# Sum of squares through Gram matrices in a fused attention and two-layer network kernel

## The chip, the cores and the metric

The kernel runs on one core of one Trainium2 chip. The metric is the time of one execution on the device in microseconds, the median of three runs: 1582.67 us before the change (1582.47 to 1583.47).

## What is computed

Three stages follow one another, all in float32.

```
p_packed = sm_attn(p, k, v)                    # 32 packed rows per head attend to 576 keys
attn     = sm_attn(q, p_packed, p_packed)      # 576 tokens per head attend to the 32 packed rows
x        = attn as (4608 tokens, 512)
rms      = sqrt(mean(x * x, axis=-1) + 1e-6);  xn = x / rms * rms_g
y        = (silu(xn @ w_gate) * (xn @ w_val)) @ w_out          # 512 -> 1536 -> 512
out      = prelu(y @ w_in, alpha) @ w_out2                     # 512 -> 2048 -> 512
```

There are 8 batches with 8 heads of 64 dimensions. A token's row of x has 512 numbers, 64 from each head; what the change concerns is the mean of their squares.

## The kernel before

**Two large stages.** Stage A does the attention and the first layer, one batch after another, each in two halves of 288 tokens; stage B does the second layer in nine tiles of 512 tokens. Every main product is written as three passes (high by high, low by high, high by low part), on operands split into a high part that TensorE multiplies quickly (fp32r) and a rest.

**The fold.** x is never built for the first layer. The probabilities a2 (32 packed rows of four heads on 128 partitions, times two groups e, times 288 tokens) are multiplied with m, the packed values already multiplied into the gate and value weights. Making m for a batch takes six "folds" (`folded`, L709): products of the packed values with the weights into two PSUM banks, whose high part ScalarE copies out (m_hi, L937) and whose rest VectorE subtracts (m_lo, L1146). In the first batch some folds go through a raw copy (L931) and GpSimd splits them (`split_m`, L502).

**The norm.** The root of the mean square is needed per token. The kernel before builds x for it: `tokens_out` (L649) has four groups x0 to x3 per batch, two for each half, each of four matmuls in 32x64 tiles of the array (L673), writing two banks. ScalarE squares a group out of PSUM (L909). In the first batch four accumulating products with a constant matrix give the mean (L682); in the other batches GpSimd adds the four squares (L484, L486) and one product per half gives it (L688). VectorE copies the mean out and adds epsilon (L1116), ScalarE takes logarithm and exponential (`rsqrt`, L912, which loads a table first, and the following silu loads another), VectorE does a Newton step of three instructions (L1124 to L1129), and a2 is multiplied with the result (`normed`, GpSimd; in the first batch `normed0`, VectorE). The two halves do this one after the other. `split` then makes an_hi and an_lo from a2.

**The order.** A half of a batch on TensorE is a loop over 12 chunks f of 128 hidden units: gate product (6 matmuls), value product (6), and, two chunks behind, `down` (12). Gate and value have one PSUM bank each, so the gate of f+1 waits for silu of f (ScalarE, L972), the value of f+1 for the product of f (VectorE, L1188); h_hi (ScalarE, L978) and h_lo (VectorE, L1191) feed `down`. All work for the batch that comes next lies between these: three tables PE_PLACES, DVE_PLACES and ACT_PLACES say at which (half, place, f) each piece stands in the fixed order of its engine. The places of TensorE are "ready" (ahead of the last three matmuls of value f; waits of the piece are put here), "after" (behind value f), "ready_down" (ahead of the last three of `down`) and "between" (behind `down`). On the other engines they are "within" (ahead of the product of f), "after" (behind it) and "between" (behind h_hi or h_lo). The tables *_FIRST hold what is left of batch 0 and runs in the first half tile. Banks 2 and 3 are shared by scores, x groups, means and folds in the batches from 1 on, so each of them waits until the one before it has been read.

**The start.** Before the first tile the pieces of batch 0 run in the order of a list at the end of each engine's program, with filler products (`keep_busy`, L804) that write nothing of use where TensorE would stand still. SP issues the loads: gv (four blocks, gate and value weights) and ow (three blocks, the output weights).

Of the kernel before, what the change touches and what calls it, by code (L numbers as in the profile page):

```python
# [73 lines left out]
}  # L74
PE_FIRST = {
    (0, "after", 3): ["x2"], (0, "between", 3): ["x3"], (0, "between", 4): ["mean1"],
# [3 lines left out]
    (0, "within", 5): ["mean1"], (0, "between", 7): ["newton1", "normed1"], (0, "within", 10): ["split1"],  # L80
}
ACT_FIRST = {
    (0, "after", 0): ["fold5"], (0, "after", 3): ["x2"], (0, "between", 3): ["x3"],
    (0, "between", 6): ["rsqrt1"], (0, "within", 9): ["split1"],
# [4 lines left out]
           "fold5": (1, LATE_BANK)}  # L89
# [4 lines left out]
def build(nc, q_t, k_t, v_s, p_t, w1_gv, w1_o, w2, rms_g, alpha, out_t):  # L94
# [3 lines left out]
    with ExitStack() as ctx:  # L98
# [42 lines left out]
        newton = place("newton", [P, HALF])  # L141
# [98 lines left out]
        def sq_of(c):  # L240
            return sq_0 if first(c) else sq
# [13 lines left out]
        def mean_ps(c, h):  # L255

            return psum[:, 1 if first(c) and h == 0 else 3, 0:HALF]

        def x_bank(c, i):

            return 0 if first(c) and i == 0 else 2

        def m_bank(c, j):

            return [4, 6, 4, 6, 2, 4][j] if first(c) else 2
# [41 lines left out]
        s2_mm, x_mm, mean_mm, m_mm = sem("s2_mm"), sem("x_mm"), sem("mean_mm"), sem("m_mm")  # L307
# [9 lines left out]
        squared, sq_part, mean_copied = sem("squared"), sem("sq_part"), sem("mean_copied")  # L317
# [39 lines left out]
        def _(sp):  # L357
# [96 lines left out]
        def _(pool):  # L454
# [7 lines left out]
            pool.wait_ge(consts_set, 3)  # L462
            nc.gpsimd.memset(v_sb[0:LAST, CHUNKS - 1, :], 0.0).then_inc(consts_set, 1)
# [17 lines left out]
            def squares(c, h):  # L481
                n = 4 * (c - 1) + 2 * h
                pool.wait_ge(squared, 4 * c + 2 * h + 2)
                nc.gpsimd.tensor_tensor(sq[:, 0:2, :], sq[:, 0:2, :], sq[:, 2:4, :], ALU.add).then_inc(sq_part, 1)  # L484
                pool.wait_ge(sq_part, n + 1)
                nc.gpsimd.tensor_tensor(sq[:, 0, :], sq[:, 0, :], sq[:, 1, :], ALU.add).then_inc(sq_part, 1)  # L486

            def normed(c, h):
                pool.wait_ge(newton_step, 6 * c + 3 * h + 3)
                nc.gpsimd.tensor_tensor(a2[:, h], a2[:, h], rinv[:, h, :].unsqueeze(1).to_broadcast([P, GROUPS, HALF]),  # L490
                                        ALU.mult).then_inc(a2n_done, 1)
# [10 lines left out]
            def split_m(j):  # L502

                n = SPLIT_BY_POOL[j]
                blocks = slice(2 * j, 2 * j + 2)
                pool.wait_ge(m_raw_done, n)
                nc.gpsimd.tensor_copy(m_hi[:, blocks], m_raw[:, blocks]).then_inc(m_part, 1)
                pool.wait_ge(m_part, n)
                nc.gpsimd.tensor_tensor(m_lo[:, blocks], m_raw[:, blocks], m_hi[:, blocks].bitcast(F32),
                                        ALU.subtract).then_inc(m_split, 1)  # L510
# [20 lines left out]
            for c in range(1, BATCH):  # L531
                scaled(c)
                squares(c, 0)
                normed(c, 0)
                squares(c, 1)
                normed(c, 1)
# [27 lines left out]
        def _(pe):  # L564
# [6 lines left out]
            def scores_ready(c, h):  # L571

                pe.wait_ge(k_in[h], 16 * (c + 1))
                if h == 0:
                    pe.wait_ge(p_in, 16 * (c + 1))
                    if c == 1:

                        pe.wait_ge(m_raw_done, 2)
                    elif c > 1:
                        pe.wait_ge(mean_copied, 2 * c)  # L580
# [50 lines left out]
            def tokens_ready(c, h):  # L631
# [4 lines left out]
                else:  # L636
                    pe.wait_ge(s2_turned, 4 * c + 2)

            def tokens(c, h):

                q = q0_sb if first(c) else q_sb
                for pair in range(PAIRS):
# [6 lines left out]
            def tokens_out(c, i):  # L649

                h = i // 2
                if i % 2 == 0:
                    pe.wait_ge(a2_turned, 2 * c + h + 1)
                if first(c):
                    if i == 1:
                        pe.wait_ge(s2_turned, 4)
                    if i == 2:
                        pe.wait_ge(scores_out, 2)
                    if i == 3:
                        pe.wait_ge(squared, 3)  # L660
                elif i == 0:
                    pe.wait_ge(m_lo_done, evicted(c) + 2)
                elif i == 1:
                    pe.wait_ge(m_lo_done, evicted(c) + 4)
                elif i == 2:
                    pe.wait_ge(mean_copied, 2 * c + 1)
                else:
                    pe.wait_ge(m_lo_done, evicted(c) + 8)
                for k in range(2):
                    pair = 2 * (i % 2) + k  # L670
                    keys = slice(PACK * pair, PACK * (pair + 1))
                    for e in range(2):
                        mm = nc.tensor.matmul(psum[HEAD_DIM * e:HEAD_DIM * (e + 1), x_bank(c, i) + k, 0:HALF],  # L673
                                              pp[keys, e, :], a2[keys, h, e, :], start=True, stop=True)
                mm.then_inc(x_mm, 1)

            def mean(c, h):

                if first(c):
                    for pair in range(PAIRS):  # L680
                        pe.wait_ge(squared, 1 + pair // 2 if h == 0 else 4)
                        mm = nc.tensor.matmul(mean_ps(c, h), mean_w[:], sq_0[:, pair, :], start=pair == 0,  # L682
                                              stop=pair == PAIRS - 1)
                    mm.then_inc(mean_mm, 1)
                else:
                    pe.wait_ge(m_lo_done, evicted(c) + 6 + 4 * h)
                    pe.wait_ge(sq_part, 4 * (c - 1) + 2 * h + 2)
                    nc.tensor.matmul(mean_ps(c, h), mean_w[:], sq[:, 0, :], start=True, stop=True).then_inc(mean_mm, 1)  # L688

            def fold_ready(c, j):  # L690
# [3 lines left out]
                if first(c):  # L694
                    pe.wait_ge(gv_in[(2 * j + 1) * W1_GROUPS // NF1], 16)
                    if j in (2, 3):
                        pe.wait_ge(m_lo_done, 2 * (j - 1))
                    if j == 4:
                        pe.wait_ge(squared, 2)
# [4 lines left out]
                elif j < 5:  # L704
                    pe.wait_ge(squared, 4 * c + j)
                else:
                    pe.wait_ge(mean_copied, 2 * c + 2)
# [12 lines left out]
            def beside(c, name):  # L720
# [17 lines left out]
                if name[0] == "x":  # L738
                    tokens_out(c, int(name[1:]))
                if name in ("mean0", "mean1"):  # L740
                    mean(c, int(name[-1]))
                if name[:4] == "fold":
# [17 lines left out]
            def tile(b, half, at):  # L760
                n = 2 * b + half
                for f in range(NF1 + LAG):
                    if f < NF1:
                        if f == 0:
                            pe.wait_ge(an_lo_done, n + 1)
                        if half == 0 and b == 0 and f // 2 in SPLIT_BY_POOL:
                            pe.wait_ge(m_split, SPLIT_BY_POOL[f // 2])
# [21 lines left out]
                    if f >= LAG:  # L789
                        d = f - LAG  # L790
                        if n == 0 and d == 0:
                            pe.wait_ge(m_lo_done, 2 * len(SPLIT_AS_USUAL))
                            pe.wait_ge(m_raw_done, len(SPLIT_BY_POOL))
# [468 lines left out]
```

## Time and profile before

| | |
|---|---|
| median of three runs | 1582.67 us |
| profiled execution | 1583.42 us, span 1581.6 us |
| TensorE busy | 1561.9 us (99%) |
| VectorE, ScalarE, GpSimd busy | 733.2, 487.4, 211.4 us |
| mean granted clock | 0.998 of full speed |

The span runs from the first to the last instruction of the profiled execution. A matmul's row shows start and duration; matmuls are pipelined, so what one costs is the distance between starts and not its duration. A product in plain float32 appears as two rows (two passes), so x16 of a group means eight matmuls. Stage A fills the first half of the span, stage B the rest.

### The profile page before, as it was taken

Reading aid. Unit: us, or ns where it says so; the run is one execution under the profiler, and the core shown is the slowest. Engines: PE = TensorE matmul, PEld = TensorE weight load, DVE = VectorE, ACT = ScalarE, POOL = GpSimd, SP = SyncE. Lnnn points to the kernel's source line nnn. Section 1 sums busy time; section 2 is a strip of 40 time slices with the busy share of each in tenths; the row PEclk is TensorE's granted clock in tenths of the full one; section 3 lists DMA queues with packets and bytes.
Section 4 is the critical chain, followed back from the end, with each engine's and each line's share of the span. In section 5 each row is a group of like instructions: output and inputs, shape, how many; then the busy total and the mean of one; then the engine's idle time right before and its main releaser. Section 6 shows DMA issues by size and latency. Waiting matters only on the chain.

```text
span 1581.6 us, 25864 instructions
## 1 busy us (share of the span) xinstructions
PE 1561.9 (99%) x10396; PEld 1319.7 (83%) x10396; DVE 733.2 (46%) x1259; ACT 487.4 (31%) x909; POOL 211.4 (13%) x149
## 2 busy tenths in 40 slices
PE   8999999999999999999999999999999999999998
PEld 3888889888897988889988888888888888888887
DVE  4655544545545455454553434343433434343343
ACT  4446354554544546352211111111111111111111
POOL 2611010000101001015570101010100101010000
PEclk9999999999999999999999999999999999999999
DMA  9212103021120212003120101010000001010000
GB/s 353 75 43 78 46 1 108 16 78 46 49 73 4 77 46 76 16 1 148 55 110 0 53 0 53 0 53 0 27 27 27 27 0 53 0 53 0 27 1 27
DMA packets 42739, 76.18 MB, mean 48 GB/s; under 512 B 2208, under 2 KB 19616, under 8 KB 42656
## 3 DMA queue, kind: packets, MB, share of 16 engines
q1 hardware_dynamic: 37472, 65.55, 12.1%
q10 hardware_dynamic: 5184, 9.44, 1.5%
q8 instruction: 62, 1.02, 0.3%
q14 instruction: 21, 0.17, 0.0%
HBM read 56.11 MB, written 18.87 MB: 47 GB/s over the span
## 4 chain that ended last, share of the span: by engine, by line
PE 93%; DVE 4%; ACT 1%; issue 1%; ACTq 0%; POOL 0%; DVEq 0%; POOLq 0%
PE psum L567 29%; PE psum L568 28%; PE psum L569 28%; PE psum L715 2%; PE psum L673 1%; DVE h_lo L1191 1%; DVE act_sb L1188 1%; PE psum L591 1%; PE psum L807 1%; ACT h_hi L978 1%; DVE m_lo L1146 1%; PE psum L605 1%; PE psum L620 1%; PE psum L645 1%; PE psum L688 0%
## 5 line engine op out<-in xcount | busy, mean ns | idle before, releaser
L1224 DVE TENSOR_TENSOR h_lo<-g,h_hi 128x512 fp32r<-128x512 f32 x144 | 126.7, 880 | 450.9 <-ACT h_hi L1005 450.9
L1005 ACT CAST h_hi<-g 128x512 fp32r<-128x512 f32 x144 | 89.4, 621 | 637.2 <-PE psum L569 566.5
L567 PE MATMUL psum<-an_hi,m_hi 128*128 128x288 f32 x768 | 236.8, 308 | 4.7 <-DVE act_sb L1188 4.5
L567 PE MATMUL psum<-h_hi,ow_hi 128*128 128x288 f32 x768 | 236.1, 307 | 0.9 <-DVE h_lo L1191 0.9
L568 PE MATMUL psum<-h_hi,ow_lo 128*128 128x288 f32 x768 | 227.2, 296 | 0.0
L568 PE MATMUL psum<-an_hi,m_lo 128*128 128x288 f32 x768 | 226.7, 295 | 0.0
L569 PE MATMUL psum<-h_lo,ow_hi 128*128 128x288 f32 x768 | 225.8, 294 | 0.0
L569 PE MATMUL psum<-an_lo,m_hi 128*128 128x288 f32 x768 | 225.7, 294 | 0.0
L567 PEld LDWEIGHTS psum<-an_hi,m_hi 128*128 128x128 f32 x768 | 144.0, 187 | 38.5 <-issue 28.5
L567 PEld LDWEIGHTS psum<-h_hi,ow_hi 128*128 128x128 f32 x768 | 144.1, 188 | 36.3 <-issue 34.6
L1188 DVE TENSOR_TENSOR act_sb<-act_sb,psum 128x288 f32<-128x288 f32 x192 | 86.8, 452 | 180.3 <-PE psum L569 170.6
L1191 DVE TENSOR_TENSOR h_lo<-act_sb,h_hi 128x288 fp32r<-128x288 f32 x192 | 107.2, 559 | 101.3 <-ACT h_hi L978 100.7
L568 PEld LDWEIGHTS psum<-h_hi,ow_lo 128*128 128x128 f32 x768 | 144.6, 188 | 0.4
L568 PEld LDWEIGHTS psum<-an_hi,m_lo 128*128 128x128 f32 x768 | 144.4, 188 | 0.4
L569 PEld LDWEIGHTS psum<-h_lo,ow_hi 128*128 128x128 f32 x768 | 144.5, 188 | 0.0
L569 PEld LDWEIGHTS psum<-an_lo,m_hi 128*128 128x128 f32 x768 | 144.3, 188 | 0.0
L567 PE MATMUL psum<-xs,w_hi_front 128*128 (+1 forms) x360 | 140.1, 389 | 0.5 <-ACT y_sb L988 0.5
L567 PE MATMUL psum<-h_hi,w_hi_front 128*128 128x512 f32 x360 | 140.6, 391 | 0.0
L568 PE MATMUL psum<-h_hi,w_lo_front 128*128 128x512 f32 x360 | 140.1, 389 | 0.0
L569 PE MATMUL psum<-h_lo,w_hi_front 128*128 128x512 f32 x360 | 140.1, 389 | 0.0
L569 PE MATMUL psum<-xs,w_hi_front 128*128 (+1 forms) x360 | 140.0, 389 | 0.0
L568 PE MATMUL psum<-xs,w_lo_front 128*128 (+1 forms) x360 | 140.0, 389 | 0.0
(137 smaller groups left out, 2428.8 us busy)
## 6 DMA issues: line engine op xcount, KB each, us to landing
k_sb<-k_t SPq DMA_DIRECT2D x16, 576.0 KB, 5.0
q_sb<-q_t SPq DMA_DIRECT2D x8, 1152.0 KB, 6.3
y_mid<-y_sb SPq DMA_DIRECT2D x16, 576.0 KB, 3.5
xs_raw<-y_mid SPq DMA_DIRECT2D x9, 1024.0 KB, 5.2
out_t<-o_sb ACTq DMA_DIRECT2D x36, 256.0 KB, 2.0
v_sb<-v_s SPq DMA_DIRECT2D x8, 1024.0 KB, 6.6
gv_sb<-w_gv SPq DMA_DIRECT2D x4, 1536.0 KB, 18.7
w_raw_front<-w SPq DMA_DIRECT2D x2, 2560.0 KB, 13.0
```

The costliest lines, as they stand in the source:

```text
L567: nc.tensor.matmul(dst, w_hi, hi, start=start, stop=False)
L568: nc.tensor.matmul(dst, w_lo, hi, start=False, stop=False)
L569: return nc.tensor.matmul(dst, w_hi, lo, start=False, stop=stop)
L591: mm = nc.tensor.matmul(dst, p_sb[dims, pair, :], k_sb[dims, pair, h * HALF:(h + 1) * HALF], start=True, stop=True)
L605: mm = nc.tensor.transpose(at_ps(c, t)[:, at:at + P], a_sb[:, g, KEY_STARTS[j]:KEY_STARTS[j] + P], ident[:])
L620: mm = nc.tensor.matmul(pp_ps[PACK * pair:PACK * (pair + 1), e * HEAD_DIM:(e + 1) * HEAD_DIM], a_t[:, j, col:col + PACK], v_sb[:, j, head ...
L645: mm = nc.tensor.matmul(s2_ps(e)[PACK * pair:PACK * (pair + 1), :], pp_t[dims, pair, :], q[dims, pair, h * HALF:(h + 1) * HALF], start=Tru ...
L715: mm = nc.tensor.matmul(psum[keys, m_bank(c, j) + e, :].rearrange("p (f n) -> p f n", f=2), pp_tg[dims, pair, :], gv_sb[dims, 2 * j:2 * j ...
L1005: nc.scalar.copy(h2_hi[:, f % 2, :], g32[:, f % 2, :]).then_inc(g_hi_done, 1)
L1188: nc.vector.tensor_tensor(act_sb[:, s, :], act_sb[:, s, :], val_ps, ALU.mult).then_inc(h32_done, 1)
L1191: nc.vector.tensor_tensor(h_lo[:, s, :], act_sb[:, s, :], h_hi[:, s, :].bitcast(F32), ALU.subtract).then_inc(h_lo_done, 1)
L1224: nc.vector.tensor_tensor(h2_lo[:, s, :], g32[:, s, :], h2_hi[:, s, :].bitcast(F32), ALU.subtract).then_inc(g_lo_done, 1)
```

## The change

The mean square of a token is a quadratic form of its probabilities: for each head, a' G a with G the 32x32 product of the packed values with themselves. The change computes these Gram matrices (eight small matmuls per batch, ahead of the token scores), VectorE multiplies them with a mask `own` that keeps the blocks of a head (`gram`), TensorE multiplies the block matrix with a2 in full-size products (v, two per half), VectorE multiplies v with a2 and adds the two groups (`weigh`), and one product with the constant matrix per half gives the mean. The two means, the root and the Newton step of both halves are done together in batches 1 to 7. ScalarE's squares and GpSimd's additions go. Folds 2 to 5 move to other places. At the start the last gv block is loaded ahead of the first ow block, fold4 of batch 0 moves into the first tile, GpSimd splits raw folds in two pieces each, and there are fillers ahead of fold1 and gram0.

```diff
 PE_PLACES = {
-    (1, "ready", 1): ["fold0_ready"], (1, "after", 1): ["fold0"], (1, "between", 2): ["x0"],
-    (1, "ready", 3): ["fold1_ready"], (1, "after", 3): ["fold1"], (1, "between", 4): ["x1"],
-    (1, "ready", 5): ["fold2_ready"], (1, "after", 5): ["fold2"], (1, "between", 6): ["mean0"],
-    (1, "after", 7): ["x2"], (1, "ready_down", 7): ["fold3_ready"], (1, "between", 7): ["fold3"],
-    (1, "after", 9): ["x3"], (1, "ready_down", 9): ["fold4_ready"], (1, "between", 9): ["fold4"],
-    (1, "after", 11): ["mean1"], (1, "ready_down", 11): ["fold5_ready"], (1, "between", 11): ["fold5"],
+    (1, "ready", 1): ["fold0_ready"], (1, "after", 1): ["fold0"], (1, "between", 2): ["gram0"],
+    (1, "ready", 3): ["fold1_ready"], (1, "after", 3): ["fold1"], (1, "between", 4): ["gram1"],
+    (1, "between", 5): ["means"], (1, "ready_down", 6): ["fold2_ready"], (1, "between", 6): ["fold2"],
+    (1, "ready", 8): ["fold3_ready"], (1, "after", 8): ["fold3"],
+    (1, "ready", 10): ["fold4_ready"], (1, "after", 10): ["fold4"],
+    (1, "ready_down", 11): ["fold5_ready"], (1, "between", 11): ["fold5"],
 DVE_PLACES = {
-    (0, "between", 8): ["turn_s0"], (0, "after", 9): ["shift0"], (0, "between", 9): ["turn_s1"],
+    (0, "between", 8): ["turn_s0", "gram"], (0, "after", 9): ["shift0"], (0, "between", 9): ["turn_s1"],
-    (1, "between", 2): ["sums1"], (1, "after", 3): ["probs1"], (1, "between", 3): ["fold1"],
-    (1, "after", 4): ["turn_p1"],
+    (1, "between", 2): ["sums1", "weigh0"], (1, "after", 3): ["probs1"], (1, "between", 3): ["fold1"],
+    (1, "after", 4): ["turn_p1"], (1, "between", 4): ["weigh1"],
+    (1, "within", 6): ["means"], (1, "between", 6): ["fold2"], (1, "between", 7): ["newton"],
 ACT_PLACES = {
+    (1, "between", 1): ["fold0"], (1, "between", 3): ["fold1"], (1, "after", 6): ["rsqrt"], (1, "between", 6): ["fold2"],
+    (1, "between", 8): ["fold3"], (1, "between", 9): ["split0"], (1, "between", 10): ["fold4"], (1, "between", 11): ["fold5"],
 PE_FIRST = {
-    (0, "after", 3): ["x2"], (0, "between", 3): ["x3"], (0, "between", 4): ["mean1"],
+    (0, "ready", 0): ["fold4_ready"], (0, "after", 0): ["fold4"], (0, "after", 3): ["gram1"], (0, "after", 4): ["mean1"],
 DVE_FIRST = {
+    (0, "between", 3): ["weigh1"], (0, "within", 5): ["mean1"], (0, "between", 7): ["newton1", "normed1"],
...
+           "fold1": (2, LATE_BANK), "gram0": (1, LATE_BANK), "fold5": (1, LATE_BANK)}
...
-            for n in range(W1_GROUPS - 1):
+            for n in range(W1_GROUPS):
                 load_gv(n)
             load_ow(0)
-            load_gv(W1_GROUPS - 1)
...
             def tokens(c, h):
+                if h == 0:
+                    for pair in range(PAIRS):
+                        for e in range(2):
+                            dims = slice(HEAD_DIM * e, HEAD_DIM * (e + 1))
+                            mm = nc.tensor.matmul(psum[PACK * pair:PACK * (pair + 1), 2 + e, HALF:HALF + PACK],
+                                                  pp_t[dims, pair, :], pp_t[dims, pair, :], start=True, stop=True)
+                    mm.then_inc(gram_mm, 1)
...
+            def gram(c, h):                                   # TensorE
+                pe.wait_ge(a2_turned, 2 * c + h + 1)
+                if first(c) and h == 1:
+                    pe.wait_ge(scores_out, 2)
+                elif not first(c):
+                    pe.wait_ge(m_lo_done, evicted(c) + 2 + 2 * h)
+                for e in range(2):
+                    mm = nc.tensor.matmul(psum[:, gram_bank(c, h) + e, 0:HALF], gram_sb[:, e, :], a2[:, h, e, :],
+                                          start=True, stop=True)
+                mm.then_inc(v_mm, 1)
...
             def fold_ready(c, j):
+                elif j == 1:
+                    pe.wait_ge(weighed, 2 * c + 1)
+                elif j == 2:
+                    pe.wait_ge(mean_copied, 2 * c + 2)
                 else:
-                    pe.wait_ge(mean_copied, 2 * c + 2)
+                    pe.wait_ge(m_lo_done, evicted(c) + 2 * j)
...
+            def gram(c):                                      # VectorE
+                dve.wait_ge(gram_mm, c + 1)
+                reached(dve, v_mm, 2 * c)
+                for e in range(2):
+                    within = psum[:, 2 + e, HALF:HALF + PACK].unsqueeze(1).to_broadcast([P, PAIRS, PACK])
+                    nc.vector.tensor_tensor(gram_sb[:, e, :].rearrange("p (q k) -> p q k", q=PAIRS), within, own[:],
+                                            ALU.mult).then_inc(gram_set, 1)
+            def weigh(c, h):
+                n = 2 * c + h + 1
+                w, bank = sq_of(c)[:, h], gram_bank(c, h)
+                dve.wait_ge(v_mm, n)
+                nc.vector.tensor_tensor(w, psum[:, bank:bank + 2, 0:HALF], a2[:, h], ALU.mult).then_inc(weighed, 1)
+                dve.wait_ge(weighed, n)
+                nc.vector.tensor_tensor(w[:, 0, :], w[:, 0, :], w[:, 1, :], ALU.add).then_inc(w_summed, 1)
```

## Rows read from the trace of the kernel before

**Rows 1.** The page: busy time of each engine, granted clock in 40 slices.
```profile
PE 1561.9 (99%) x10396; PEld 1319.7 (83%) x10396; DVE 733.2 (46%) x1259; ACT 487.4 (31%) x909; POOL 211.4 (13%) x149
...
PEclk9999999999999999999999999999999999999999
```
**Rows 2.** TensorE's waits from 75 to 1040 us: total, times, longest.
```profile
PE psum L567 <- DVE act_sb L1188: 3.4, 9, 1.2
PE psum L673 <- DVE m_lo L1146: 1.8, 7, 0.3
```
**Rows 3.** Timeline around an x group: start, duration, instruction.
```profile
106.03 0.29 PE L569 MATMUL psum<-h_lo,ow_hi 128*128 128x288 f32 x1
106.25 0.71 PE L673 MATMUL psum<-a,pp 32*64 32x288 f32 x8
...
107.13 0.29 PE L568 MATMUL psum<-an_hi,m_lo 128*128 128x288 f32 x1
```
**Rows 4.** Timeline around a mean product.
```profile
114.46 0.30 PE L569 MATMUL psum<-h_lo,ow_hi 128*128 128x288 f32 x1
114.60 0.65 PE L688 MATMUL psum<-sq,mean_w 128*128 128x288 f32 x2
...
115.21 0.29 PE L568 MATMUL psum<-an_hi,m_lo 128*128 128x288 f32 x1
```
**Rows 5.** TensorE at the start: the packed values' products.
```profile
15.40 1.32 PE L620 MATMUL psum<-v_sb,a_t 128*32 128x64 f32 x80
```
**Rows 6.** VectorE in batch 2's preparation, half 1, f=2 to 3.
```profile
191.87 1.25 DVE L1146 TENSOR_TENSOR m_lo<-psum,m_hi 128x512 fp32r<-128x512 f32 x2
193.04 0.44 DVE L1188 TENSOR_TENSOR act_sb<-act_sb,psum 128x288 f32<-128x288 f32 x1
...
195.34 0.27 DVE L1100 RECIPROCAL rcp<-sum 128x18 f32<-128x18 f32 x1
...
196.25 0.75 DVE L1105 TENSOR_TENSOR e<-e,rcp 128x576 f32<-128x576 f32 x1
```
**Rows 7.** TensorE in batch 2's preparation: x0 to the fold's ready point in value 3.
```profile
193.27 0.71 PE L673 MATMUL psum<-a,pp 32*64 32x288 f32 x8 [0.26 <-DVE m_lo L1146]
...
195.21 0.29 PE L567 MATMUL psum<-an_hi,m_hi 128*128 128x288 f32 x1
```
**Rows 8.** ScalarE around one half's root.
```profile
215.99 1.06 ACT L937 CAST m_hi<-psum 128x512 fp32r<-128x512 f32 x2
217.06 1.28 ACT L972 ACT_TABLE_LOAD   x1
```
**Rows 9.** The start: VectorE and TensorE.
```profile
16.79 0.29 DVE L1070 COPY pp<-psum 128x128 f32<-128x128 f32 x1 [1.67 <-PE psum L620]
...
25.60 1.27 PE L673 MATMUL psum<-a,pp 32*64 32x288 f32 x16 [1.61 <-DVE a L1110]
...
27.60 3.91 PE L682 MATMUL psum<-sq,mean_w 128*128 128x288 f32 x8 [0.74 <-ACT sq L909]
...
31.55 0.46 DVE L1116 TENSOR_SCALAR mean<-psum 128x288 f32<-128x288 f32 x1 [3.58 <-PE psum L682]
...
36.78 0.40 PE L567 MATMUL psum<-an_hi,m_hi 128*128 128x288 f32 x1
```
**Rows 10.** Busy time per engine (PE, PEld, DVE, ACT, POOL), clock, DMA, GB/s.
```profile
20.00:25.00 5.00, 2.06 (x40) 0.37 (x32) 4.79 (x10) 2.55 (x5) 0.00 (x0) 0.93 1.01 404
25.00:27.00 2.00, 1.27 (x16) 0.34 (x16) 2.00 (x4) 0.27 (x2) 0.65 (x1) 0.50 1.04 390
```
**Rows 11.** First tile: ScalarE, GpSimd, VectorE, TensorE.
```profile
47.49 0.65 ACT L909 ACTIVATE sq<-psum 128x576 f32<-128x576 f32 x1 [0.71 <-PE psum L673]
...
53.89 2.46 POOL L509 TENSOR_TENSOR m_lo<-m_raw,m_hi 128x1024 fp32r<-128x1024 f32 x1
...
54.42 2.24 DVE L1058 TENSOR_SCALAR a_sb<-a_sb,rcp 128x576 f32<-128x576 f32 x1
...
59.32 0.85 PE L605 MATMUL psum<-ident,a_sb 128*128 128x128 f32 x6 [1.18 <-DVE mean L1116]
```

More of the change, by code:

```diff
@@ L140, in build @@
         a2 = place("a2", [P, 2, GROUPS, HALF])
-        newton = place("newton", [P, HALF])
+        gram_sb = place("gram_sb", [P, 2, P])
+        own = place("own", [P, PAIRS, PACK])
         p_sb = place("p_sb", [P, PAIRS, PACK])
@@ L240, in sq_of @@
         def sq_of(c):
-            return sq_0 if first(c) else sq
+            return (sq_0 if first(c) else sq)[:].rearrange("p (h e) n -> p h e n", e=2)
         def mean_of(c):
@@ L647, in tokens @@
                 mm.then_inc(s2_mm, 1)
[L649 to L675, printed above, removed]
@@ L690, in fold_ready @@
+            def mean(c, h):
+                pe.wait_ge(w_summed, 2 * c + (h + 1 if first(c) else 2))
+                nc.tensor.matmul(mean_ps(c, h), mean_w[:], sq_of(c)[:, h, 0, :], start=True, stop=True).then_inc(mean_mm, 1)
             def fold_ready(c, j):
@@ L737, in beside @@
                     tokens(c, int(name[-1]))
-                if name[0] == "x":
-                    tokens_out(c, int(name[1:]))
+                if name in ("gram0", "gram1"):
+                    gram(c, int(name[-1]))
                 if name in ("mean0", "mean1"):
                     mean(c, int(name[-1]))
+                if name == "means":
+                    mean(c, 0)
+                    mean(c, 1)
                 if name[:4] == "fold":
@@ L811, in _ @@
             for name in ("scores0", "scores1", "turn_a01", "turn_a2", "packed", "turn_packed", "tokens0", "fold0", "tokens1",
-                         "fold1", "x0", "x1", "mean0", "fold2", "fold3", "fold4", "fold5"):
+                         "fold1", "gram0", "mean0", "fold2", "fold3", "fold5"):
                 if name in FILLERS:
@@ L927, in folded @@
             def folded(c, j):
-                act.wait_ge(m_mm, NF1 // 2 * c + j + 1)
-                if first(c) and j in SPLIT_BY_POOL:
+                act.wait_ge(m_mm, FIRST_M[j] if first(c) else NF1 // 2 * c + j + 1)
+                if first(c) and j in RAW_M:
                     bank = m_bank(c, j)
@@ L991, in _ @@
             nc.scalar.preload_act_table_set("natural_log_exp_and_others")
-            for name in ("exp0", "exp1", "turn_a0", "turn_a2", "packed", "probs0", "fold0", "fold1", "x0", "x1", "probs1",
-                         "rsqrt0", "silu", "fold2", "split0", "fold3", "fold4"):
+            for name in ("exp0", "exp1", "turn_a0", "turn_a2", "packed", "probs0", "fold0", "fold1", "probs1",
+                         "rsqrt0", "silu", "fold2", "split0", "fold3", "fold5"):
                 beside(0, name)
@@ new lines, in weigh, with mean @@
+            def weigh(c, h):
[5 more added lines that the diff above has]
+                nc.vector.tensor_tensor(w[:, 0, :], w[:, 0, :], w[:, 1, :], ALU.add).then_inc(w_summed, 1)
+            def mean(c, halves):
+                dve.wait_ge(mean_mm, 2 * c + halves.stop)
+                if first(c):
+                    src = mean_ps(c, halves.start).unsqueeze(1)
+                else:
+                    dve.wait_ge(a2_turned, 2 * c + 2)
+                    src = psum[:, 2:4, 0:HALF]
+                nc.vector.tensor_scalar(mean_of(c)[:, halves, :], src, 0.0, RMS_EPS, ALU.max,
+                                        ALU.add).then_inc(mean_copied, halves.stop - halves.start)
@@ L1122, in newton_of @@
+            def newton_of(c, halves):
+                n = 3 * halves.start if first(c) else 3 * c + 3
+                root, whole, part = rinv_of(c)[:, halves, :], mean_of(c)[:, halves, :], sq_of(c)[:, halves, 1, :]
                 reached(dve, newton_step, n)
-                dve.wait_ge(rsqrt_done, 2 * c + h + 1)
-                nc.vector.scalar_tensor_tensor(out=newton[:], in0=mean_of(c)[:, h, :], scalar=-0.5, in1=root,
+                dve.wait_ge(rsqrt_done, n // 3 + 1)
+                nc.vector.scalar_tensor_tensor(out=part, in0=whole, scalar=-0.5, in1=root,
@@ L1169, in beside @@
                     turn_p(c, int(name[-1]))
+                if name == "gram":
+                    gram(c)
+                if name in ("weigh0", "weigh1"):
+                    weigh(c, int(name[-1]))
                 if name in ("mean0", "mean1"):
-                    mean(c, int(name[-1]))
+                    mean(c, slice(int(name[-1]), int(name[-1]) + 1))
+                if name == "means":
+                    mean(c, slice(0, 2))
                 if name in ("newton0", "newton1"):
-                    newton_of(c, int(name[-1]))
+                    newton_of(c, slice(int(name[-1]), int(name[-1]) + 1))
+                if name == "newton":
+                    newton_of(c, slice(0, 2))
                 if name in ("split0", "split1"):
@@ L1202, in _ @@
             dve.wait_ge(consts_set, 4)
-            for name in ("max0", "max1", "norm0", "norm1", "turn_a1", "packed", "turn_s0", "shift0", "turn_s1", "sums0",
-                         "probs0", "turn_p0", "shift1", "fold0", "fold1e0", "mean0", "fold1e1", "newton0", "normed0",
-                         "split0"):
+            for name in ("max0", "max1", "norm0", "norm1", "turn_a1", "packed", "turn_s0", "gram", "shift0", "turn_s1",
+                         "sums0", "probs0", "turn_p0", "shift1", "weigh0", "fold0e0", "mean0", "fold0e1", "newton0",
+                         "normed0", "fold1e0", "split0", "fold1e1"):
                 beside(0, name)
```

127 lines of the change are left out of this document (50 added, 77 removed), and 6 rows, old and new, of tables (ACT_PLACES, DVE_PLACES).

## The prediction

> **What bounds the kernel now.** I read the page's first two parts first: TensorE is busy for 99% of the span and its granted clock is at full speed in all forty slices [rows 1]. So the time is TensorE's instruction stream, and an edit is worth what it takes out of that stream or out of TensorE's waits. The waits come second: between 75 and 1040 us, in 965 us, TensorE idles 3.4 us for the gate-times-value product and 1.8 us for the first fold's low part; the second is 0.26 us in each of seven batches [rows 2]. No shorter wait in those 965 us can give much. The removed work must be found in the timeline, and every added wait must be looked for there.
>
> **The change in the steady batches (1 to 7).** They are alike, so I work out one and multiply by seven. Before, each has four x groups of four tiled matmuls, and two mean products.
> An x group: the last ordinary matmul ahead of it starts at 106.03, the second one behind it at 107.13. Without the group these would be two steps of 0.13 us apart, so a group costs 1.10 - 0.26 = 0.84 us [rows 3]. A full 128x128 f32 product over 288 columns: 114.46 to 115.21 less two steps is 0.48 us [rows 4]. The two mean products only move next to each other: 0.96 before and after.
> Removed: groups x2 and x3, 2 x 0.84 = -1.68. Groups x0 and x1 become two full products each, 0.96 for 0.84: +0.12 each. By TensorE work alone that is -1.44 a batch, -10.1 us in all.
> Tiny Gram products: eight matmuls of 32 columns, two passes each, in the tile shape of the token scores that follow them. The nearest row has 80 passes of 64 columns in 1.32 us, 0.0165 each [rows 5]: 16 x 0.0165 = 0.26. Issue and columns may hide behind the scores that follow in the same shape, so 0.05 is the lower end (a fifth of that), 0.40 the upper (half as much again). I take 0.2. The Trainium skill's page "TensorE: Matmul & The Clock Gate", section "Part 1: The HAM clock gate", says that starts of successive matmuls are never nearer than about 25 ns however few columns they have. By that rule the group takes 0.40 us and seven batches 1.4 us more than by my value; the 80 passes of [rows 5] are nearer together than that, so the row decides.
>
> **The wait that it adds.** In half 1 fold1 writes banks 2 and 3, in which v0 now lies, so fold1 must wait until VectorE has weighed v0. Before, ScalarE read x0 at once and this wait was free. VectorE is a strict chain here: low part of fold0 until 193.12, product of f=2, low part of h, the sums, whose reciprocal ends at 195.34 + 0.27 = 195.61, and only then the product of f=3 [rows 6]. The change puts weigh0 behind the sums. It is a 128x576 product with one operand in PSUM; a 128x576 one takes 0.75, a 128x288 one from PSUM 0.44 [rows 6], so 0.75, and "weighed" comes at 196.37. This moment doesn't depend on TensorE.
> TensorE: x0 waits for the low part and starts at 193.27, and the matmul behind the fold's ready point starts at 195.21 [rows 7]. Between them lie x0 (0.84 less the 0.10 lead) and nine matmuls, 0.13 apart. With v0: 193.27 + 0.96 + 9 x 0.13 = 195.4. The weighing releases it at 196.37, and a released group starts 0.15 later (193.12 to 193.27): 196.52. So there is a **new wait of some 1.1 us**, and this mark moves by 196.52 - 195.21 = +1.31, v0's own +0.12 being in it.
> Behind the waiting matmul stand the second half of value 3, fold1, down1; all move with it. VectorE adds the two rows (0.44) inside that time and is then waiting for TensorE, as now.
> Batch: +1.31 (x0 to v0 with the wait) + 0.12 (v1) - 1.68 (x2, x3) + 0.2 (Gram) = **-0.05 us**, seven batches -0.35. Bounds: weigh0 as short as 0.65 or as long as 0.85, Gram 0.05 to 0.40, and up to 0.3 of new small waits behind: -0.3 to +0.5 a batch, -2 to +3.5 us in seven.
>
> What else could wait in such a batch, each with its cover. v1 needs turn_p1, which is 0.45 + 0.77 behind the product of f=4, against down2's 1.58: some 0.2 to spare. The joint root stands on ScalarE between silu and h_hi of f=6: table load 1.28, two functions at most 0.75 each, h_hi, fold2's two copies of some 1.07 together, another load of 1.28 [rows 8]; silu of f=7 then ends 0.2 before gate 8 wants it. If that cover is gone, each 0.1 of lateness costs 0.7 in all. Newton on 576 elements is 3 x 0.75 = 2.25 at once in place of twice 3 x 0.45; the product of f=8 waits for it, value 9 is 1 us later still. In half 0 the two mask products (128x128, a copy of which takes 0.29 [rows 9], so 0.6) stand before tokens1; TensorE comes there 1.0 after turn_s0. GpSimd loses the squares, which hid anyway.
>
> **The start.** The chain is now turn_p0 until 25.55, x0/x1 at 25.60, squares, eight passes of the mean from 27.60 to 31.5 at half the clock, mean copy at 31.55, root, norm, split, first main matmul at 36.78: 5.23 us behind the mean copy [rows 9]. The clock is granted at 0.50 in 25 to 27 us, that is 1.2 GHz, after TensorE had been idle for much of 20 to 25 [rows 10]. After the change: mask products and Gram +0.7 on the chain, so turn_p0 at 26.25; v0 1.15, weigh0 0.75, add 0.45, one mean product 0.65 and hand-overs: mean copy at 29.55 if the clock stays up. The second half's exponential and the table load put the root not before 30.25 where the mean copy alone would let it start at 30.0; so the first main matmul comes at about 35.0, **-1.8**. The extra fillers before fold1 and gram0 keep TensorE busier in 21 to 26 us; if the clock is at 1.2 GHz all the same, v0 and the mean cost 1.4 more: -0.4. Reordered loads: the last gv block no longer comes behind 1 MB of ow, so it is not what fold5 waits for; ow comes some 3 us later, but is used first at f=2, 41 us. The low part of fold1 and the fold4 taken into tile 0 need 0.65 and 1.22 us, both beside that first tile.
>
> **First tile, half 0.** VectorE is the chain: ScalarE's square of x2 (0.65 at 47.49) stands before the exponentials, VectorE's second norm takes 2.24 because it starts inside GpSimd's 2.46 us subtraction, and the transposes of TensorE wait until 59.32 [rows 11]. Changes on this chain: x2 off ScalarE -1.35 (with the load behind it), weigh1 +1.2, half-size GpSimd pieces: a hold of at most 1.3 in place of 2.4, on average -0.6. From -1.8 this gives -2.5 at 59.32, between -4 and +1. TensorE's own work (fold4 in, x2, x3 and three of four mean products out: -0.9) hides in its wait. Tokens1 of batch 1 already waits for VectorE; the mask products and Gram add 0.6: -1.9.
> That hold is what the Trainium skill's page "SBUF — State Buffer", section "SBUF: two separate sides", calls an exclusive lock on a port pair that VectorE and GpSimd share: who starts second stands still for the whole instruction. If both norms fell outside GpSimd's pieces the rule would give 1.2 more of gain, if the adds of weigh1 fell in, as much less; both lie in the bounds above.
>
> **Sum.** -1.9 - 0.35 = -2.2. The profiled execution took 1583.42 (span 1581.6 and 1.8 around it), the median is 1582.67, 0.75 below; the differences are the same: 1582.67 - 2.2 = **1580.5**.
>
> **Rivals.** (A) The new wait is not there or is short, because weigh0 comes out earlier than I put it: then each batch gives 1.1 more: -2.2 - 7.5 = -9.7, **1573**. For: the whole TensorE work falls by 10 us. Against: the order on VectorE in [rows 6] leaves no room before 195.61. (B) The time gets longer: besides the wait at fold1, silu of f=7 misses gate 8. It has 0.2 to spare, and decides from there; with the joint root late by 0.9 us (a mean copy that comes late behind the product, longer functions) it costs 0.7 in each of seven batches, +4.9: **1585.4**. Against: the mean is ready 1.7 us before the root can start. (C) The start loses its gain, the clock dropping at the beginning of tile 0: 4 us at half clock cost 2 us and the 1.8 is gone: -0.35 + 0.6 + 1.5 = +1.8: **1584.4**. For: [rows 10], and TensorE still idles between v0 and the mean. (D) The half-batches do what the text says but fold1's wait is partly given back, half of it: **1576.5**.
>
> **Chances.** Forecast 0.52, A 0.10, D 0.17, B 0.08, C 0.13. 0.2% is 3.2 us, about what a measurement tells from no change. Faster by more: A, D and the lower end of the forecast, 0.36; slower by more: B, 0.07; within: 0.57. The range from 1574.5 to 1584.5 leaves out A and B.
>
> **What would show it.** A wait of TensorE at value 3 for weigh0, about 1.1 us seven times, is the step on which most hangs; its absence means A. v groups at 0.96, no x groups; mask products of 0.3; no wait for silu at gate 8; first main matmul at 35.0; transposes of tile 0 at 56.8; distance between batches changed by less than 0.5 us. A distance shorter by over 1 us would prove the forecast wrong.

## The result, and the profile after

The changed kernel is slower: 1593.99 us, median of 4 runs (1591.07 to 1594.44), against 1583.07 us before (4 runs, 1582.47 to 1584.8). The ratio is 1.0063, with a 95% interval of 1.0046 to 1.0081. The forecast was 1580.5 us, with a range from 1574.5 to 1584.5. The profiled execution below is the fastest of the four; the other three took 1593.57 to 1594.44 us.

The page of the profiled execution (1591.07 us, span 1589.3) answers to [rows 1]: TensorE is as full as before and its clock is up in all slices.

```profile
PE 1566.7 (99%) x10326; PEld 1323.5 (83%) x10326; DVE 750.1 (47%) x1279; ACT 447.7 (28%) x849; POOL 183.5 (12%) x132
...
PEclk9999999999999999999999999999999999999999
```

70 rows fewer on TensorE, and yet 4.8 us more of busy time. So the first question is in which stage the time lies. The first product on `xs` divides the two stages; it starts at 792.9 us before and at 785.6 after:

| | before | after | |
|---|---|---|---|
| stage A (all that was edited) | 792.9 | 785.6 | -7.3 |
| stage B (no line edited) | 788.7 | 803.7 | +15.0 |

**Stage A did what it was made for, and more than I forecast. Stage B, which has not one changed instruction, takes it back twice over.** (The 7.3 us are those of one execution; e1 below, with the same instructions at other addresses, has 6.3.) Stage B is nine tiles of 384 products of 128x128 by 512 columns, 3456 in all; +15.0 us is 4.3 ns on each. The same stretch of 200 us in stage B (length, busy time and number of matmuls of TensorE, clock, DMA share, GB/s), before:

```profile
1000.00:1200.00 200.00, 200.00 (x883) 1.00 0.06 21
```

and after:

```profile
1000.00:1200.00 200.00, 200.00 (x866) 1.00 0.06 21
```

TensorE is never idle in either, the clock is full in both, DMA is the same; it gets 17 products fewer through. The groups by line tell which ones (busy time, mean ns of one). Before, in 1000 to 1180 us:

```profile
L567 PE MATMUL psum<-h_hi,w_hi_front 128*128 128x512 f32 x85 | 33.2, 391 | 0.0
L568 PE MATMUL psum<-xs,w_lo_front 128*128 x84 | 32.7, 389 | 0.0
...
L567 PE MATMUL psum<-xs,w_hi_back 128*128 x16 | 6.2, 389 | 0.0
```

After:

```profile
L567 PE MATMUL psum<-xs,w_lo_front 128*128 x84 | 33.2, 395 | 0.0
...
L566 PE MATMUL psum<-h_hi,w_hi_front 128*128 128x512 f32 x81 | 32.0, 395 | 0.0
...
L566 PE MATMUL psum<-xs,w_hi_back 128*128 x16 | 6.2, 389 | 0.0
```

The products on the front part of w2 (10 of 16 chunks, so 2160 of the 3456 products) are those that take longer. The starts in the traces say it more exactly. Over the whole of stage B a front product is followed by the next start after 226.8 ns on average before and after 232.9 ns in the changed kernel. Some products on the mid and back parts are slowed too, where they stand right behind a group on the front part. If all +15.0 us is put on the 2160 front products, it is 6.9 ns on each.

The front part begins where gv_sb did, at byte 17696, in both kernels. What lies behind the first edited line here does not stand still:

```diff
-        newton = place("newton", [P, HALF])
+        gram_sb = place("gram_sb", [P, 2, P])
+        own = place("own", [P, PAIRS, PACK])
         p_sb = place("p_sb", [P, PAIRS, PACK])
```

`place` gives out addresses in SBUF one behind the other. `newton` (1152 B) went, `gram_sb` (1024 B) and `own` (512 B) came, so m, ow, an, h and, on top of them, xs, h2 and the mid and back parts of w2 lie 384 B higher (xs 104992 to 105376). xs holds the tokens and h2 the hidden values that stream through TensorE in stage B (the moving operands); the parts of w2 are the weights. The traces name h2 as h_hi and h_lo.

### The profile page after: what moved, and what is told of

Read it like the earlier page. It is cut to its first block, busy times and chain, and to the rows that moved or that the text cites. A ratio compares the mean times of both kernels' runs of the same rounds, so it can differ in the third digit from the quotient of the medians.

```text
span 1589.3 us, 25626 instructions
## 1 busy us (share of the span) xinstructions
PE 1566.7 (99%) x10326; PEld 1323.5 (83%) x10326; DVE 750.1 (47%) x1279; ACT 447.7 (28%) x849; POOL 183.5 (12%) x132
## 4 chain that ended last, share of the span: by engine, by line
PE 91%; DVE 4%; ACT 1%; issue 1%; DMA 1%; SPq 0%; ACTq 0%; DVEq 0%
PE psum L566 29%; PE psum L567 28%; PE psum L568 28%; PE psum L698 3%; DMA gv_sb<-w_gv 1%; DVE h_lo L1197 1%; DVE act_sb L1194 1%; ACT h_hi L956 1%; DVE sum L1072 1%; DVE m_lo L1144 1%; PE psum L586 1%; PE psum L600 0%; PE psum L660 0%; PE psum L648 0%; PE psum L667 0%
## 5 line engine op out<-in xcount | busy, mean ns | idle before, releaser
L567 PE MATMUL psum<-an_hi,m_lo 128*128 128x288 f32 x768 | 226.7, 295 | 0.0
L1197 DVE TENSOR_TENSOR h_lo<-act_sb,h_hi 128x288 fp32r<-128x288 f32 x192 | 110.7, 576 | 115.4 <-ACT h_hi L956 115.4
L566 PE MATMUL psum<-xs,w_hi_front 128*128 (+1 forms) x360 | 142.4, 395 | 0.5 <-ACT y_sb L966 0.5
L568 PE MATMUL psum<-xs,w_hi_front 128*128 (+1 forms) x360 | 142.1, 395 | 0.0
```

What stands on the lines that cost most here:

```text
L566: nc.tensor.matmul(dst, w_hi, hi, start=start, stop=False)
L567: nc.tensor.matmul(dst, w_lo, hi, start=False, stop=False)
L568: return nc.tensor.matmul(dst, w_hi, lo, start=False, stop=stop)
L1197: nc.vector.tensor_tensor(h_lo[:, s, :], act_sb[:, s, :], h_hi[:, s, :].bitcast(F32), ALU.subtract).then_inc(h_lo_done, 1)
```

## The experiments

Each row of this table is one kernel; "shifted" says by how many bytes the moving operands were moved against the front weights, compared with before. Stage B is read from the profile. The kernel before ran again beside each set of experiments (medians 1582.73 to 1583.31 us), and the ratios are to those runs.

| kernel | shifted | stage B | time, median | ratio to before, 95% interval |
|---|---|---|---|---|
| before | - | 788.7 | 1583.07 | |
| after | all behind p_sb +384 | 803.7 | 1593.99 | 1.0063 [1.0046, 1.0081] |
| e1 after, old addresses | 0 | 788.7 | 1578.01 | 0.9969 [0.9957, 0.9981] |
| e2 before, shifted | +384 | 803.0 | 1597.91 | 1.0092 [1.0077, 1.0108] |
| e3 e1 and weigh0 first | 0 | 788.7 | 1572.35 | 0.9927 [0.9913, 0.9941] |
| e4 e1 and old loads | 0 | 788.7 | 1579.23 | 0.9974 [0.9963, 0.9984] |
| e5 from e3 | -32 | 802.8 | 1588.56 | 1.0028 [1.0012, 1.0044] |
| e6 from e3 | +128 | 803.8 | 1587.03 | 1.0025 [1.0014, 1.0037] |
| e7 from e3 | +256 | 788.8 | 1571.35 | 0.9923 [0.9901, 0.9946] |
| e8 from e3 | only h2, +384 | 800.6 | 1583.58 | 1.0000 [0.9989, 1.0011] |
| e9 e3, no new fillers | 0 | 788.7 | 1573.60 | 0.9939 [0.9924, 0.9954] |
| e10 e3, mean1 later | 0 | 788.7 | 1571.48 | 0.9929 [0.9915, 0.9943] |
| e11 from e3 | weights too, +128 | 788.7 | 1571.83 | 0.9929 [0.9910, 0.9947] |
| e12 from e3 | stage A's an, act, h +128 | 788.7 | 1573.78 | 0.9941 [0.9919, 0.9964] |

**e1: the changed kernel at the old addresses.**

```diff
-        own = place("own", [P, PAIRS, PACK])
+        place("gap", [P, 32])
...
         sq_0 = place("sq_0", [P, PAIRS, HALF], at=y_at)
+        own = place("own", [P, PAIRS, PACK])
```

> The changed kernel with the SBUF addresses of before: the mask `own` (512 B) goes behind y_sb and a gap of 128 B takes its place, so that p_sb and all that lies behind it (m, ow, an, h, xs, the mid and back parts of w2) are back at their old addresses; no instruction changes. Stage B (from the first product on xs to the end) took 788.7 us before and 803.7 after the change, though no line of it was changed, while stage A became 7.3 us shorter. Theory L (addresses): the 384 B shift of the moving operands and of part of the weights makes each 128x512 product 5 ns slower; expected here: stage B 788.7, spacing of its products 226 ns, span 1574.3, time about 1576. Rival P (place of the code): 11 instructions fewer on TensorE ahead of the loop of stage B shift it in memory; expected: stage B still 803.7, time 1591 to 1594. Rival N (noise between executions): stage B anywhere between the two.

Stage B takes 788.7 us, as theory L said, to the tenth; the time is 1578.01, 2 us more than it expected. The row of 1000 to 1200 us is that of before again:

```profile
1000.00:1200.00 200.00, 200.00 (x883) 1.00 0.06 21
```

**e2: the kernel before, 384 B of nothing put in.**

```diff
+        place("gap", [P, 96])
         p_sb = place("p_sb", [P, PAIRS, PACK])
```

> The kernel before with a gap of 384 B ahead of p_sb and nothing else: its data behind it lie at the addresses of the changed kernel. L: stage B 803.7 in place of 788.7, time 1598. P and N: no change, 1583. Stage A under L: no change expected by more than 1 us, since the changed kernel's batches fit the sum of their instructions.

Stage B takes 803.0 us, and the time is 14.6 us longer than that of the kernel before in the same set (1583.31). One unused gap makes the old kernel slower than the changed one. With e1 this is the full square: old or new code, old or new addresses; stage B follows the addresses alone. P and N fall.

**e5, e6, e7: other shifts** (`place("gap", [P, 24])`, `[P, 64]`, `[P, 96]` where e3 has `[P, 32]`).

> e3 with p_sb and all behind it 32 B lower (xs at 104960 in place of 104992; gv and so the front part of w2 stay at 17696). What decides the spacing of stage B's products is open between: distance modulo 512 B of the moving operand from the weights (theory D; the slow kernels have xs 128 B and h2 128 B above the front weights' residue of 288 modulo 512, the fast ones 256 B), and the operand's own residue (theory R; slow 416, fast 32). D: a small change, stage B within 3 us of 788.7. R: residue 0, stage B 788.7 or less.

> e3 with the same data 128 B higher: residue of xs and h2 160, distance from the front weights -128. D, if the size of the distance counts: slow like the changed kernel, stage B near 803; mid and back weights move with xs and keep their spacing. R: residue 160, somewhere between; stage B under 796.

> e3 with the same data 256 B higher: residue 288, the front weights' own, distance 0. D: if near is bad, the slowest of all, over 803; if it is the half distance of 256 that is good, over 795. R: residue 288, no reason to differ from the fast one by more than the 416 one does.

+256 is as fast as 0, and -32, +128 and +384 all cost some 14 to 15 us in stage B. D was right for +128 alone: it expected little from -32 and a slow stage from +256. R was wrong for -32 and for +128. What fits all five is the distance **modulo 256 B**: fast where it is 0, slow at 128 and at 32 B below, the only two others measured. The operands' own residue modulo 256 (32 where stage B takes 788.7 us, 0 and 160 where it takes 803) fits as well, and e11 is there to part the two.

**e8: only the second layer's hidden values.**

```diff
-        h2_at = back_at + 2 * w2_back * w2_size
+        h2_at = back_at + 2 * w2_back * w2_size + 384
-        o_sb = place("o_sb", [P, KC, TILE], at=an_at)
+        o_sb = place("o_sb", [P, KC, TILE], at=an_at + 384)
```

> e3 with only the second layer's hidden values (h2_hi, h2_lo and what lies with them, and o_sb) 384 B higher; xs and all weights as in e3. If each product's spacing goes by its own operands, the products on h2 (half of all) slow down by 5 to 6 ns where the weights are the front part and those on xs keep theirs: stage B about 788.7 + 7.5 = 796. If only xs or the weights' place counts: 788.7.

Stage B 800.6: more than the 796 expected, since now h2 is off against all weights. Product by product it is plain; in 1000 to 1180 us:

```profile
L568 PE MATMUL psum<-xs,w_lo_front 128*128 x83 | 32.4, 391 | 0.0
L569 PE MATMUL psum<-h_lo,w_hi_front 128*128 128x512 f32 x82 | 32.4, 395 | 0.0
...
L569 PE MATMUL psum<-h_lo,w_hi_back 128*128 128x512 f32 x16 | 6.3, 395 | 0.0
```

The products on h2 take 394 to 395 ns with the front and the back weights alike, those on xs with the same front weights 390 to 391, near the 389 of before. So it goes by product and not by stage. By the starts in the trace, products on h2 are 232.7 ns apart, and of the twelve products of a group on xs behind one on h2 only the first three are slow (about 231.8, 232.5 and 230.9 ns), the other nine 226.6 to 227.4: a slow group also slows the first few products behind it.

**e11: weights and data shifted together** (`place("lead", [P, 32])` ahead of gv_sb).

> e3 with everything from gv_sb on 128 B higher, so that weights and moving operands keep their distances and all residues change. So far stage B took 788.7 to 788.8 with the moving operands at distance 0 or +256 B from the front weights (modulo 256), and 803 with +384, +128 and -32. Theory D (only the distance modulo 256 B counts): 788.7. Rival R (the operands' own residue, 32 modulo 256 being good): xs, h2 and weights are at 160 modulo 256 here, stage B 803 or more.

Stage B takes 788.7 us. All residues are new, the distances old, and the time is the old one. R falls.

**e12: the same in stage A** (`place("gap2", [P, 32])` ahead of an_hi).

> e3 with an, act, h, y_sb and the mask 128 B higher and all else in place: in stage A the moving operands (an_hi, an_lo, h_hi, h_lo) are then 128 B from the residue modulo 256 that m and ow have; stage B's operands are untouched. The distance rule has so far been seen on 128x512 products only (226 to 232 ns apart). If it holds for stage A's 128x288 products too, whose weight load (188 ns) is longer than their spacing (132 ns), they come further apart by some ns: 4608 products, +5 ns would be +23 us in stage A. If the weight load alone sets their spacing or the rule needs 512 columns: stage A as in e3 (782.3 us until the first product on xs), stage B 788.7 in both.

A batch takes 94.51 us in place of 94.235 in e3 (transposes of batch 2 to 7, five distances each): +0.28 us for its 576 products, 0.5 ns on each. But this does not say that the rule spares products of 288 columns, since the premise of the experiment was wrong. The pieces of an and of h lie 288 x 4 = 1152 B apart, which is 128 modulo 256, so in e3 every other piece already is 128 B off its weights. The shift puts right those that were off and puts off those that were right: 272 of a batch's 576 products are in line in e3, 304 in e12.

The single products show it. Take the third pass of `down`, h_lo on ow_hi, by the three pieces of h, and count the mean distance from its start to the next one in the whole of stage A (distances over 160 ns left out):

| piece of h_lo | e3 | e12 |
|---|---|---|
| 0 | 130.6 ns, in line | 135.5 ns, off |
| 1 | 135.5 ns, off | 130.5 ns, in line |
| 2 | 130.0 ns, in line | 135.9 ns, off |

These 5 ns change sides with the shift. In the other passes the difference is smaller, and in some there is none, so in the sum of a batch the two nearly cancel. What stage A would gain with all pieces in line was not tried.

**e3: weigh0 ahead of the sums** in DVE_PLACES.

```diff
-    (1, "between", 2): ["sums1", "weigh0"], (1, "after", 3): ["probs1"], (1, "between", 3): ["fold1"],
+    (1, "between", 2): ["weigh0", "sums1"], (1, "after", 3): ["probs1"], (1, "between", 3): ["fold1"],
```

> e1 with weigh0 ahead of the sums of half 1 on VectorE in batches 1 to 7. In the changed kernel TensorE waits 0.6 us at value 3 for weigh0, seven times, behind sums1. Theory: the weighing then ends about 0.7 us earlier than TensorE asks for it, the wait is gone and the sums hide (product of f=3 some 0.7 later, used by value 4 only after fold1 and down1): 0.6 to 0.7 us a batch, 4.5 us less than e1. Rival: the product of f=3 or the probabilities come late and the wait moves to value 4 or to v1 behind turn_p1: gain under 1.5 us.

The wait for weigh0 is gone from the list, and e3 is 5.7 us faster than e1 by the medians, where 4.5 was expected. e1's wait lies between v0 and fold1:

```profile
191.26 1.21 PE L661 MATMUL psum<-a,gram_sb 128*128 128x288 f32 x4 [0.26 <-DVE m_lo L1145]
194.87 1.09 PE L699 MATMUL psum<-gv_sb,pp_tg 64*32 64x512 f32 x16
```

In e3:

```profile
190.95 1.21 PE L661 MATMUL psum<-a,gram_sb 128*128 128x288 f32 x4 [0.26 <-DVE m_lo L1145]
193.66 1.09 PE L699 MATMUL psum<-gv_sb,pp_tg 64*32 64x512 f32 x16
```

3.61 against 2.71: 0.90 us a batch, where the idle column says 0.61 for such a wait (its row in the changed kernel is shown below). The column counts from the modelled end of the last matmul; the starts tell the whole price. The distance between batches says the same: 95.13 in e1, 94.23 in e3.

**e4: the old order of the loads** in e1.

> e1 with the old order of the loads: first ow block ahead of the last gv block. Theory: fold5 and fold4 of batch 0 wait for the gv block until some 33.3 us as before, the first main product comes 0.5 to 1.5 us later than in e1 and the time grows by as much. Rival: the root's chain ends so late that the loads hide anyway: no difference (under 0.3 us).

The list of waits up to 80 us shows the wait coming back, where e1 has none of its kind:

```profile
PE psum L700 <- DMA gv_sb<-w_gv: 1.9, 2, 1.0
```

but it costs nothing that shows: from the first transposes (12.14 in e4, 12.90 in e1) to the first main product it takes 22.98 us in e4 and 22.83 in e1, and the intervals of the two ratios overlap. The rival was right: whether the loads are reordered or not, they hide.

**e9: e3 without the fillers ahead of fold1 and gram0.**

> e3 without the fillers ahead of fold1 and gram0, which the change had added. Theory: without them TensorE's clock is granted at 1.2 GHz from about 24 to 31 us as in the kernel before; v0 and the mean product take 0.96 us more and 0.48 us more, the first main product comes 1 to 2 us later and the time is 1 to 2 us longer. Rival: the chain over VectorE and ScalarE hides it, under 0.5 us. A clock that stays up without them would say that the fillers do nothing.

e9 in 20 to 25 and 25 to 30 us (columns as in [rows 10]):

```profile
20.00:25.00 5.00, 2.03 (x35) 0.40 (x32) 4.83 (x12) 2.55 (x5) 0.00 (x0) 0.85 1.02 408
25.00:30.00 5.00, 3.05 (x6) 1.67 (x6) 3.00 (x5) 2.13 (x3) 1.16 (x1) 0.50 1.02 403
```

e3:

```profile
20.00:25.00 5.00, 4.55 (x38) 1.37 (x38) 4.83 (x11) 2.44 (x5) 0.00 (x0) 1.00 1.03 410
25.00:30.00 5.00, 2.15 (x8) 1.01 (x8) 3.88 (x7) 2.86 (x5) 1.16 (x1) 1.00 1.01 397
```

TensorE was busy for 2.03 of 5 us without the fillers, 4.55 with them, and the clock is granted at half in 25 to 30 us (1.2 GHz) without, at full (2.4 GHz) with them. The first main product comes at 38.34 against 35.59, the transposes of the first tile at 60.25 against 58.23: 2.0 us. By the medians it is 1.25 us, and in the two profiles all of stage A differs by 0.6; the intervals of the two ratios meet, so the gain of the whole is not as sure as the clock.

**e10: mean1 of batch 0 behind down2.**

> e3 with the first batch's second mean product behind down2 of the first tile (as before the change) in place of ahead of it. In e3 TensorE waits 1.8 to 1.9 us there for weigh1, with down2 (1.6 us) standing behind. Theory: down2 runs in that wait; but VectorE's mean copy and with it the transposes move only as far as the product comes earlier or later, so a part of the 1.6 us is seen as a longer wait at value 5: 0.3 to 1.2 us less than e3. Rival: VectorE alone sets the transposes' time: no gain (under 0.2).

TensorE's waits for the weighing up to 80 us fall from 3.3 to 2.3 us in two waits, and 1.1 for the product of f=4 and 1.2 of the transposes for the mean copy come in their place. From the first main product to those transposes it takes 22.78 us in e10 and 22.64 in e3. The medians are 1571.48 and 1572.35, intervals overlapping: a gain under 1 us, if there is one, and by the trace the rival is nearer. e7, e10, e11 and e3 are all about 0.7% faster than before and beat both kernels.

## Why the prediction was wrong

**The step that failed** is **the sum**, "-1.9 - 0.35 = -2.2": it adds up changes in stage A only and so takes stage B, whose instructions the diff doesn't touch, to cost what it did. That term was put at nothing without a reason. The change has three lines of `place`, and I read them as names. They moved both moving operands of stage B by 384 B against the front weights. e1 and e2 show the price of that alone, +15.0 us (803.7 - 788.7) and +14.3 (803.0 - 788.7), and none of my rivals had it. Why the chip is slower with such a distance stays open.

Without it the time is e1's, 1578.01: between my forecast and rival D, and inside the range. That is in part luck, since the terms inside the sum were off too: my batches gained too little, and the end of stage A, which I took at nothing, gained 2.4 us in e1.

Term by term, on stage A:

- **A batch.** Forecast -0.05 us, measured -0.35: the distance of the transposes of batches 2 to 7 is 95.49 before and 95.14 after. That is just outside my bound of -0.3. The mechanism and the place were right, two sizes were not. In the changed kernel, TensorE at value 3:

```profile
189.06 1.21 PE L660 MATMUL psum<-a,gram_sb 128*128 128x288 f32 x4 [0.25 <-DVE m_lo L1144]
...
191.17 0.30 PE L568 MATMUL psum<-an_lo,m_hi 128*128 128x288 f32 x1
192.07 0.40 PE L566 MATMUL psum<-an_hi,m_hi 128*128 128x288 f32 x1 [0.61 <-DVE sq L1102]
```

 and VectorE:

```profile
191.14 0.27 DVE L1076 RECIPROCAL rcp<-sum 128x18 f32<-128x18 f32 x1
191.33 0.69 DVE L1102 TENSOR_TENSOR sq<-psum,a 128x576 f32<-128x576 f32 x1
192.06 0.46 DVE L1104 TENSOR_TENSOR sq<-sq 128x288 f32<-128x288 f32 x1
```

 weigh0 starts 0.19 behind the reciprocal's start, not 0.27, and takes 0.69, not 0.75. The matmul starts are 0.90 apart for an ordinary 0.13, so the wait costs 0.77 and not 1.1. Up to this mark x0 and v0 with their waits take 192.07 + 0.10 - 188.52 = 3.65 against 195.21 - 192.71 = 2.50 before: +1.15 (forecast +1.31). (188.52 and 192.71 are the starts of down0's last product; the 0.10 is there because the matmul that waited is followed after 0.24 and not 0.13.)
- **Tiny Gram products.** Forecast 0.2. The last product ahead and the second one behind the scores:

```profile
164.16 0.29 PE L568 MATMUL psum<-an_lo,m_hi 128*128 128x288 f32 x1
164.39 0.27 PE L642 MATMUL psum<-pp_t 64*32 64x32 f32 x13
...
165.34 0.30 PE L567 MATMUL psum<-h_hi,ow_lo 128*128 128x288 f32 x1
```

 1.18 with them; before, 1.11 for the scores alone (168.43 to 169.54). So 0.07: near the lower end that I gave. By the floor of about 25 ns between starts, which the prediction quotes from the Trainium skill's page "TensorE: Matmul & The Clock Gate", section "Part 1: The HAM clock gate", they would have cost 0.40. The trace does not agree: eight of these passes start within 47 ns (164.389 to 164.436), some 7 ns apart. With 0.07 and +1.15: 1.15 + 0.12 - 1.68 + 0.07 = -0.34, the measured -0.35.
- **The joint root.** Right: it is late for nobody. Both functions take 0.69 and 0.68 (bound 0.75); no wait of TensorE names silu. Rival B did not happen.
- **The start.** Forecast -1.8 for the first main product; it starts at 33.24 (36.78 before) in the changed kernel's profile, where the clock stayed up from 25 to 35 us, and at 35.73 in e1's, where it was granted at 0.66 of full in 30 to 35. The two differ in no instruction. So -3.5 or -1.05. Of the 2.5 us between them 0.9 is there already at the first transposes (11.96 and 12.90). From those to the first main product it takes 21.28 and 22.83 us; these 1.6 us come together with the lower clock, so rival C's cause is real. The old kernel spreads as much: 23.49 us in its profile and 25.41 in e2's.
- **The first tile.** Forecast: transposes at 56.8; measured 55.42, e1 57.64. The wait at mean1 for weigh1, 1.8 us, was not in my list; VectorE's chain hid it, as e10 shows.
- **Tokens1 of batch 1.** The 0.6 us wait for the mask product is there (0.2 before).
- **The end of stage A**, which I took as unchanged: from the last transposes to the first product on xs 159.1 us before (159.3 in e2), 157.8 after and 156.7 in e1 and e4, a gain of 1.3 to 2.4 us; with e3's order it is 155.7 to 157.1. About 0.35 of it is a batch's usual gain, and the rest fits TensorE's waits for the product of f in this stretch: 2.1 us before, 1.1 after, 0.2 in e1. Before, VectorE's h_lo takes 2.23 us in place of 0.46 at 754.21, beside one of GpSimd's first splits of w2 (753.73 to 756.12). Whether such a hold is met less often by chance or because of the squares that GpSimd no longer has was not tried.

Sum for e1: 1.7 (to the transposes) + 0.4 (first batch) + 5 x 0.35 + 2.4 (end) = 6.3 = 792.9 - 786.6.

## What to carry to other kernels

When a diff adds or takes away a buffer, work out the addresses of all that lies behind it, and compare the distance of moving operand and weights of every large product modulo 256 B with the old one. Do this for every piece of a buffer: pieces 1152 B apart, as here, take turns at being in line. A gap of a few bytes is the cheapest of all experiments. When a change of one stage is judged, measure the time of each stage apart, and look at the spacing of untouched instructions before looking for a cause in the touched ones. On an engine that works down a fixed list, whatever reads the bank that TensorE waits for goes ahead of what nobody waits for.

## What the runs showed of the hardware

- The next product starts 226.7 to 227.0 ns after a 128x128 by 512 product with fp32r operands where its moving operand and its weights lie at the same residue modulo 256 B in SBUF (before, e1, e3, e7, e11), and 232.7 to 233.2 ns after it, as a mean over the products on the front weights, where they don't (after, e2, e5, e6; distances of 32 B below and 128 B above measured). The first few products behind a slow group are slowed too. Stage B gets 14 to 15 us longer by it. Absolute addresses play no part (e11). Why, no run here shows, nor whether it is the product's own weights or those of the next one that count.
- With 288 columns the third pass of `down` is followed after 130.0 to 130.6 ns in line and 135.5 to 135.9 ns off (e3, e12); other passes differ less or not at all.
- TensorE's busy share, the clock and the DMA rows of stage B were the same in all these kernels; only the mean duration (389 and 395 ns) and the count in 200 us (883 or 884, and 865 to 867) told of it.
- Eight tiny products (64x32 by 32 columns) ahead of eight of the same tile shape cost 0.07 us in all.
